# Splitting most of the weights during the first group, with GpSimd for the low parts of the first four pieces

## The reference

```python
# 1. attention with decay: batch 4, 8 heads, 768 tokens, head size 48
cur = einsum('bhd,bhe->bhde', u * kt, vt)
y[:, :, t] = einsum('bhd,bhde->bhe', rt, state + cur)
state = w * state + einsum('bhd,bhe->bhde', kt, vt)
# 2. gated layer on x: 3072 tokens x 384, hidden size 1536
x = (sigmoid(x @ w_gate) * (x @ w_val)) @ w_out
# 3. each token goes to one of 8 experts (hidden size 1024)
logits = normalised(x) @ normalised(expert_emb).T / tau
e = argmax(logits);  out = softmax(logits)[e] * (relu(x @ w1[e]) @ w2[e])
```

## Time and profile before

| what | value |
|---|---|
| median of 3 runs | 874.27 us (873.17 to 874.39) |
| the profiled execution's own time | 874.71 us |
| its span, first to last instruction | 873.0 us |
| TensorE busy (matmul) | 846.8 us, 97% of the span |
| VectorE, ScalarE, GpSimd busy | 430.7, 303.2, 426.2 us |
| 0 to 16 us | TensorE busy 11.22 of 16.00, mean clock 0.89 |
| 16 to 55.6 us | TensorE busy 32.02 of 39.60, mean clock 0.68 |
| 55.6 to 128.8 us (group 0) | TensorE busy 73.09 of 73.20, mean clock 0.96 |
| 128.8 to 196 us | TensorE busy 67.20 of 67.20, mean clock 1.00 |

### The profile page before, as it was taken

One profiled execution on the slowest core, in us unless ns is written; L12 is line 12 of the kernel. 1 busy time (PEld: TensorE's weight loads), 2 busy tenths in 40 slices (PEclk: granted clock), 3 DMA queues, 4 the chain that ended last, 5 costly groups with the idle time before them and its releaser, 6 DMA issues.

```text
span 873.0 us, 20522 instructions
## 1 busy us (share of the span) xinstructions
PE 846.8 (97%) x7508; PEld 798.4 (91%) x7509; DVE 430.7 (49%) x1051; ACT 303.2 (35%) x622; POOL 426.2 (49%) x452
## 2 busy tenths in 40 slices
PE   7799999999999999999999999998999999999995
PEld 6689999999999999999999999987899989989995
DVE  6755456456446446445545542386356266265100
ACT  1532232233233233223223223423544444454442
POOL 3656417417417417416516513245566476466544
PEclk8869999999999999999999999999999999999999
DMA  9532202302302212212212200236344344354110
GB/s 279 198 117 76 84 29 84 93 21 85 88 26 84 71 43 85 78 35 84 71 41 87 65 33 19 73 108 174 111 142 144 114 150 143 101 159 138 50 35 29
DMA packets 76021, 79.68 MB, mean 91 GB/s; under 512 B 5720, under 2 KB 73248, under 8 KB 75952
## 3 DMA queue, kind: packets, MB, share of 16 engines
q1 hardware_dynamic: 62800, 57.93, 22.0%
q10 hardware_dynamic: 9216, 9.55, 3.9%
q0 software_dynamic: 3936, 11.23, 3.4%
HBM read 67.47 MB, written 12.01 MB: 91 GB/s over the span
## 4 chain that ended last, share of the span: by engine, by line
PE 89%; DVE 5%; POOL 2%; issue 2%; DMA 1%; ACT 1%; SPq 0%; POOLq 0%; ACTq 0%; DVEq 0%
PE ps L1261 35%; PE ps L1278 17%; PE ps L1374 13%; PE ps L1359 13%; PE ps L1382 3%; PE ps L1187 2%; PE ps L1210 1%; PE ps L1194 1%; PE ps L1218 1%; PE ps L1339 1%; PE ps L1224 1%; POOL weights L626 1%; DMA staged<-in_moe_w 1%; DVE weights L1015 1%; DMA w_col<-in_w 0%
## 5 line engine op out<-in xcount | busy, mean ns | idle before, releaser
L1261 PE MATMUL ps<-x_groups,weights 128*128 128x384 f32 x1728 | 317.9, 340 | 0.0
L1261 PEld LDWEIGHTS ps<-x_groups,weights 128*128 128x128 f32 x1728 | 299.9, 189 | 1.9
L567 POOL TENSOR_TENSOR hT<-gate,hT 128x384 fp32r<-128x384 f32 x96 | 104.3, 1089 | 138.4 <-ACT hT L705 138.4
L1278 PE MATMUL ps<-weights,hT 128*128 128x392 f32 x864 | 160.6, 344 | 0.0
L1278 PEld LDWEIGHTS ps<-weights,hT 128*128 128x128 f32 x864 | 152.6, 188 | 0.4
L1374 PE MATMUL ps<-weights,hT 128*128 x672 | 124.1, 339 | 1.7 <-ACT h_f L807 1.7
L1359 PE MATMUL ps<-weights,x_groups 128*128 (+1 forms) x504 | 122.8, 397 | 1.2 <-DVEq L1020 1.0
L1027 DVE TENSOR_TENSOR gate<-ps,gate 128x384 f32<-128x384 f32 x96 | 53.6, 558 | 136.8 <-PE ps L1261 130.3
L1374 PEld LDWEIGHTS ps<-weights,hT 128*128 128x128 f32 x672 | 115.9, 188 | 1.9 <-issue 1.9
L1359 PEld LDWEIGHTS ps<-weights,x_groups 128*128 128x128 f32 x504 | 92.6, 188 | 20.4 <-issue 1.7
L1013 DVE CAST weights<-staged 128x768 fp32r<-128x768 f32 x56 | 50.3, 898 | 102.2 <-PE ps L1359 55.1
(11 more groups left out here) (181 smaller groups left out, 1001.9 us busy)
## 6 DMA issues: line engine op xcount, KB each, us to landing
staged<-in_moe_w SPq DMA_DIRECT2D x60, 384.0 KB
r_in<-routed ACTq DMA_DIRECT2D x30, 192.5 KB
rk_raw<-in_rt SPq DMA_DIRECT2D x21, 256.0 KB, 3.6
rk_raw<-in_kt SPq DMA_DIRECT2D x21, 256.0 KB, 3.9
r_in<-in_r SPq DMA_DIRECT2D x21, 192.0 KB, 2.4
k_in<-in_k SPq DMA_DIRECT2D x21, 192.0 KB, 2.5
v_in<-in_v SPq DMA_DIRECT2D x21, 192.0 KB, 2.3
first_raw<-in_moe_w_out SPq DMA_DIRECT2D x6, 384.0 KB, 14.0
```

What stands on the lines that cost most here:

```text
L567: g.tensor_tensor(hT_lo[:, f, :], gate[:, f % 2, :], hT_hi[:, f, :].bitcast(F32), ALU.subtract).then_inc(hlo_ready, 1)
L1261: ins = te.matmul(ps[:, bank[f % 2], 0:GT], wt[:, c, fs], x[:, half, c, :], start=(c == 0 and m == 0), stop=(c == KC - 1 and m == 2))
L1278: ins = te.matmul(ps[:, BX2[i], 0:XW], h[:, f, ts], wt[:, f, :], start=(f == 0 and m == 0), stop=(f == FC - 1 and m == 2))
```

## The change

1. The host passes a transposed w_out as one more input; six pieces t0 to t5 of it are loaded and TensorE reads the logit chunks from them directly. The transposes of w_out on TensorE and ScalarE's copies are gone. The o pieces are still loaded, so six more pieces of 384 KB are.
2. Before the first hidden step only g0, v0, g1 and v1 are split: high parts on ScalarE, low parts on GpSimd (early_lo): g0 after tile 0's attention, v0 after tile 1's, g1 and v1 after tile 2's.
3. The other 14 pieces are split in group 0, behind the hidden steps that HI_AT (ScalarE), LO_AT (VectorE) and LO_O_AT (GpSimd) name.
4. Rooms are reused: PIECES gives each piece a room, and SyncE waits until the piece that was in it is used up. The loads of tiles 3 to 5 stand between those of the pieces. ScalarE issues the inputs of tiles 0 to 2 (18 DMAs) ahead of all its other work.
5. The order of the start is written out anew, without FIRST; VectorE scales k of the next tile ahead of stage 2. GpSimd makes k_tok ahead of its wait for y_turned, in every tile.
6. In group 0, TensorE waits for g and v of a pair of steps at even f, for o pieces in the projection.

The orders in which pieces are loaded (with the room of each: s the staging buffers, h the room of h_f, x beside the first group's x, l in the second half of h) and split:

```diff
+    PIECES = [("g", 0, "s0"), ("v", 0, "s1"), ("t", 0, "l0"), ("t", 1, "l1"), ("t", 2, "l2"), ("t", 3, "x0"),
+              ("t", 4, "x1"), ("t", 5, "x2"), ("g", 1, "h"), ("v", 1, "l3"), ("g", 2, "l4"), ("v", 2, "l5"),
+              ("g", 3, "s0"), ("v", 3, "s1"), ("o", 0, "x0"), ("o", 1, "x1"), ("o", 2, "x2"), ("v", 4, "l3"),
+              ("g", 4, "h"), ("g", 5, "l4"), ("v", 5, "l5"), ("o", 3, "s0"), ("o", 4, "s1"), ("o", 5, "h")]
...
+    HI_SEQ = [("g", 0), ("v", 0), ("g", 1), ("v", 1), ("g", 2), ("o", 0), ("o", 1), ("v", 2), ("o", 2), ("g", 3),
+              ("v", 3), ("v", 4), ("o", 3), ("g", 4), ("o", 4), ("g", 5), ("v", 5), ("o", 5)]
+    LO_SEQ = [("g", 0), ("v", 0), ("g", 1), ("v", 1), ("g", 2), ("v", 2), ("g", 3), ("v", 3), ("v", 4), ("g", 4),
+              ("g", 5), ("v", 5)]
+    HI_AT = {1: "g2 o0", 2: "o1 v2", 3: "o2 g3", 4: "v3", 5: "v4 o3", 6: "g4 o4", 7: "g5", 8: "v5 o5"}
+    LO_AT = {1: "g2", 3: "v2", 4: "g3 v3", 5: "v4", 7: "g4 g5", 8: "v5"}
+    LO_O_AT = {2: "o0 o1", 3: "o2", 6: "o3 o4", 8: "o5"}
+    LO_POOL = LO_SEQ[:4]
...
+        def lo_count(kind, j):
+
+            if kind == "o":
+                return piece_done_o, j + 1
+            n = LO_SEQ.index((kind, j)) + 1
+            return (piece_done_first, n) if (kind, j) in LO_POOL else (piece_done, n - len(LO_POOL))
```

SyncE's queue; load_pieces waits until the piece before in the same room is used up:

```diff
+            load_pieces(PIECES[:17])
+            fetch(sp, 0, 3)
+            fetch_v(sp, 0, 3)
+            load_pieces(PIECES[17:20])
+            fetch(sp, 0, 4)
+            load_pieces(PIECES[20:21])
+            fetch_v(sp, 0, 4)
+            load_pieces(PIECES[21:23])
+            fetch(sp, 0, 5)
+            fetch_v(sp, 0, 5)
+            load_pieces(PIECES[23:])
```

GpSimd, in the loop over f behind attention(f - 1) and hidden_step(f), in hidden_step, and at the start behind each tile:

```diff
                     hidden_step(G, f)
+                    if G == 0:
+                        for kind, j in pieces_at(LO_O_AT, f):
+                            _, raw, hi, lo = piece(kind, j)
+                            pool.wait_ge(piece_hi, HI_SEQ.index((kind, j)) + 1)
+                            g.tensor_tensor(lo, raw, hi.bitcast(F32), ALU.subtract).then_inc(piece_done_o, 1)
...
+                if G == 0 and f in (6, 8, 10):
+                    pool.wait_ge(*lo_count(*{6: ("v", 4), 8: ("g", 5), 10: ("v", 5)}[f]))
...
+            def early_lo(kind, j):
+                _, raw, hi, lo = piece(kind, j)
+                pool.wait_ge(piece_hi, HI_SEQ.index((kind, j)) + 1)
+                g.tensor_tensor(lo, raw, hi.bitcast(F32), ALU.subtract).then_inc(piece_done_first, 1)
...
+                if i < 2:
+                    early_lo("gv"[i], 0)
+            early_lo("g", 1)
+            early_lo("v", 1)
```

ScalarE (make_hi waits for the piece to land and casts it; it also stands in the loop over f, by HI_AT) and, in its stage 3 of tile 3, a wait for o2, whose room the next group's x takes:

```diff
+                    if isinstance(T, int) and T == TPG:
+                        act.wait_ge(*lo_count("o", 2))
...
+            for c in range(TPG):
                 fetch(act, 0, c, waits=False)
                 fetch_v(act, 0, c, waits=False)
...
+            make_hi("g", 0)
+            make_hi("v", 0)
+            for i in range(TPG):
+                attention(0, i, i, 3, 0)
+            make_hi("g", 1)
+            make_hi("v", 1)
```

VectorE, in the loop over f behind attention(f - 1), and its start:

```diff
                         attention(*att_of(b, half, f - 1), 1 - half)
+                    if G == 0:
+                        for kind, j in pieces_at(LO_AT, f):
+                            make_lo(kind, j)
...
+            def make_lo(kind, j):
+                _, raw, hi, lo = piece(kind, j)
+                dve.wait_ge(piece_hi, HI_SEQ.index((kind, j)) + 1)
+                ve.tensor_tensor(lo, raw, hi.bitcast(F32), ALU.subtract).then_inc(piece_done, 1)
+
+            attention(0, 0, 0, 1, 0)
+            for i in range(TPG):
+                if i + 1 < TPG:
+                    scale_k(0, i + 1)
+                attention(0, i, i, 2, 0)
+                if i + 1 < TPG:
+                    scale_r(0, i + 1)
+                attention(0, i, i, 3, 0)
+                if i + 1 < TPG:
+                    attention(0, i + 1, i + 1, 1, 0)
```

TensorE, its hidden step and its start:

```diff
-                if f * P % GCOLS == 0:
-                    pe.wait_ge(piece_done, split_by(ORDER.index(("v", f * P // GCOLS))))
+                if G == 0 and f * P % GCOLS == 0:
+                    for kind in "gv":
+                        pe.wait_ge(*lo_count(kind, f * P // GCOLS))
...
+            for i in range(TPG):
+                attention(0, i, i, 1)
+                if i == 0:
                     turn_embeddings()
...
+                    pe.wait_ge(enT_ready, 1)
+                for c in range(4 * i, 4 * i + 2):
+                    logit_columns(c)
+                attention(0, i, i, 2)
+                for c in range(4 * i + 2, 4 * i + 4):
+                    logit_columns(c)
+                attention(0, i, i, 3)
+                keep_clock(BX2[1], 4)
             hidden_step(0, 0, 0, first=True)
```

More of the change, by code:

```diff
@@ L61, in fused_kernel @@
     NWO, NWG = FC // OCH, FF // GCOLS
-    PRE = NWO + 2 * NWG
     XH = 256
@@ L210, in fused_kernel @@
         enT_ready = sem("enT_ready")
-        first_in = [sem(f"first_in{n}") for n in range(NFIRST)]
+        room_arrived = {room: sem("arrived_" + room) for room in dict.fromkeys(ROOM_OF.values()) if room[0] != "s"}
         staged_in = [sem("staged_in0"), sem("staged_in1")]
@@ L349, in fetch_v @@
             if waits:
-                before = 1 if T == 2 else T
+                before = 1 if T == TPG else T
                 eng.wait_ge(y_psum, before)
@@ L455, in _, with load_pieces @@
                          u.rearrange("h d -> (h d)").partition_broadcast(P)).then_inc(small_in, 16)
[L457 to L463, removed]
+            def load_pieces(pieces):
+                for kind, j, _ in pieces:
+                    src, raw, _, _ = piece(kind, j)
+                    if tenant_before(kind, j) is not None:
+                        sp.wait_ge(*consumed(*tenant_before(kind, j)))
+                    sp.dma_start(raw, src).then_inc(landed(kind, j)[0], 16)
+            load_pieces(PIECES[:17])
[9 more added lines that the diff above has]
+            load_pieces(PIECES[23:])
+            for T in range(2 * TPG, NT):
                 fetch(sp, *divmod(T, TPB))
@@ L527, in attention @@
                 if stage == 0:
+                    start = isinstance(T, int) and T == 0
                     pool.wait_ge(*arrival(T))
-                    if not (isinstance(T, int) and T == 0):
-                        pool.wait_ge(y_turned, T)
+                    if start:
+                        pool.wait_ge(pow_ready, 1)
+                    else:
                         pool.wait_ge(scores, T)
-                    if isinstance(T, int) and T == 0:
+                    g.tensor_tensor(k_tok[:, :, 0:D], k_t[:, :, :], pow_tok[:, :, :], ALU.mult).then_inc(k_tok_ready, 1)
+                    if start:
                         pool.wait_ge(small_in, 48)
@@ L744, in split_first, with make_hi @@
                     s_.copy(hi, expert_view(0, i, chunks)).then_inc(piece_hi, 1)
-            for c in range(2):
+            def make_hi(kind, j):
+                _, raw, hi, _ = piece(kind, j)
+                piece_arrived(act, kind, j)
+                s_.copy(hi, raw).then_inc(piece_hi, 1)
+            for c in range(TPG):
                 fetch(act, 0, c, waits=False)
@@ L1227, in logit_columns @@
             def logit_columns(c):
-                pe.wait_ge(wo_copied, c + 1)
+                raw = piece("t", c // 2)[1]
+                if c % 2 == 0:
+                    piece_arrived(pe, "t", c // 2)
                 for q in range(KC):
-                    for part in HALVES:
-                        ins = te.matmul(ps[part, BX, c * E:(c + 1) * E], gate[:, c % 2, q * P:(q + 1) * P][:, part],
-                                        enT[:, q, :], start=(q == 0), stop=(q == KC - 1))
+                    for n, part in enumerate(HALVES):
+                        at = c % 2 * P + n * HP
+                        ins = te.matmul(ps[part, BX, c * E:(c + 1) * E], raw[:, q, at:at + HP], enT[:, q, :],
+                                        start=(q == 0), stop=(q == KC - 1))
                 ins.then_inc(wo_logit, 1)
```

204 lines of the change are left out of this document (89 added, 115 removed).

## The result

The changed kernel takes 876.38 us (median of 20 runs, 873.86 to 880.22) against 873.38 (870.76 to 877.85): 3.0 us slower, ratio 1.0034, 95% interval 1.0020 to 1.0049. The forecast was 873.6: the sum of −0.7 put to the profiled execution, less its 0.4 above the median then shown. The time lies in the stated range; its direction was given 0.35. The two profiled executions differ by less, 875.92 against 874.71, because each lies on the other side of its own median.

What follows compares the result with a forecast made beforehand. TensorE was taken to bound the kernel from 55.6 us on, GpSimd's weight splitting to pace the start. −13.7+5.4+4.8+2.8 = −0.7 us against 874.7 gave 874.0, less 0.4 for the median 873.6; range 866.5 to 879.

Steps and rivals of the forecast that it cites:

- The start, −13.7: Before group 0's first hidden step: that step starts at 41.9 instead of 55.63 us; bounds −15.5 and −10.
- so no other engine can take much of this away: Start, tile 1 to 2: GpSimd's multiply and wait are under 1 us shorter than VectorE's and TensorE's path to y.
- tile 1 to 2, 8.3: Start: masks and bonus sum 2.05, multiply 1.6, v0's low part 1.83, k_tok 1.7, matmuls 1.15, ending at 34.9.
- The first hidden step at the lower clock, no term: Group 0, first hidden step: expected at the lower clock as before, so no gain or cost.
- Step 4, +5.4 (2.4 to 6.4): Group 0: TensorE stalls before step 4 for v2's low part, behind stage 2 of tile 3 on VectorE; +5.4 us.
- Step 6, no term: Group 0: no TensorE stall priced before step 6; only VectorE's product of step 6 late, by 0.5 to 2.2, taken 1.2.
- Step 8, +4.8: Group 0: TensorE stalls before step 8 for g4's low part, behind stage 2 of tile 4; +4.8 us, bounds 2.4 and 5.8.
- Clock, +2.8: Group 0, behind the stalls before steps 4 and 8: each clock fall costs 0 to 2.9, taken 1.4; +2.8 us together.
- GpSimd is in time: Group 0: both stalls only 2.4 and too short for the clock; −8.9 us, 865; chance 0.12.
- Tile 2's inputs are late: Start: tile 2's inputs land after 28.6; at 3 us late +2.3, 876.6; chance 0.15.
- both stalls at their upper bounds and slow refill: Group 0, steps 4 and 8: stalls 12.2 together plus 5 for the clock; +3.5 us, 877.8; chance 0.13.
- rival 4: Start doesn't shorten because something else paces the tiles; counted only as part of "Tile 2's inputs are late", no own chance.

Runs made afterwards that it cites:

- vector_first_four: Changed kernel with VectorE instead of GpSimd making the low parts of g0, v0, g1 and v1; ratio 1.0031 to the kernel before.
- no_fill: Changed kernel without the clock-keeping matmuls at the end of each of the start's three tiles; 879.26 us, ratio 1.0050 to the kernel before.
- fill_stalls: Changed kernel plus 36 and 24 calls of the clock-keeping matmul before the waits of steps 4 and 8; ratio 1.0004 to the kernel before.
- lows_earlier: Changed kernel with VectorE's low parts of v2 behind step 2 (was 3) and g4 behind 6 (was 7); 868.38 us, ratio 0.9923 to before.
- w_out_spread: Changed kernel with GpSimd's low part of o1 moved from step 2 to 3 and o4 from 6 to 7; ratio 1.0011 to the kernel before.
- fill_short: Changed kernel plus 24 and 14 calls of the clock-keeping matmul before the waits of steps 4 and 8; ratio 0.9981 to the kernel before.
- low_after_scale: Changed kernel with GpSimd waiting for VectorE's scaling of the next tile's r before g0's and v0's low parts; ratio 1.0041 to the kernel before.
- one_low_spread_vector: Changed kernel with one VectorE low part a step, w_out's spread on GpSimd, VectorE making the first four; 864.37 us, ratio 0.9876 to before.

## Why the prediction was wrong

The sum was −0.7 us and +3.0 was measured (+2.0 in this pair of traces, at the end of the first group's hidden steps). The large terms held to 1.6 us or better; what turned the sign is a start 1.6 us later than worked out and a third stall of 1.6 that had no term, with step 4 at its upper bound (0.9), against 2.0 that the first step gave.
- *The start, −13.7.* Measured −12.1. The step "so no other engine can take much of this away" failed. I followed GpSimd; but in this trace TensorE's own queue is the chain of tiles 1 and 2. Per tile it holds 24 matmuls twice (L1313, the logit chunks, 1.4 us each) and eight filling ones (L1387, 1.7) among the others, all at the lower clock. Of the three terms of the start the one that failed is "tile 1 to 2, 8.3": VectorE's first mask operations of the two tiles begin 9.5 us apart, the tile before and the tile behind are within 0.2 of theirs. The chain has no GpSimd in it, and vector_first_four, which takes GpSimd's four pieces away, doesn't start sooner; no_fill, which takes 1.7 us out of TensorE's queue there, brings the 9.5 to 7.8, and fill_stalls, with the upper clock there, to 7.7. In the six other traces with this start GpSimd does come in ahead of tile 1, by another way than the one I priced: VectorE's scaling of r, which begins during GpSimd's low part of g0, takes 3.0 to 4.2 us, and TensorE waits 0.4 to 1.7 for it. VectorE's two rows, and the chain of waits through tile 1, of the changed kernel:

```profile
26.82 0.36 DVE L960 TENSOR_TENSOR A_room<-ps,Z 128x192 f32<-128x192 f32 x1 [1.89 <-PE ps L1273]
...
36.33 0.36 DVE L960 TENSOR_TENSOR A_room<-ps,Z 128x192 f32<-128x192 f32 x1 [2.56 <-PE ps L1273]
```

```profile
26.75 1.38 PE ps L1313 x24
...
32.66 1.71 PE ps L1387 x8
```

- *The first hidden step at the lower clock, no term.* It gave −2.0: 3.96 us from start to product instead of 5.97, since the upper clock came within 2 us of its start. I had expected it to run as before; this gain was not foreseen, and it hid about half of the 4.1 us of the other errors.
- *Step 4, +5.4 (2.4 to 6.4).* Measured 6.3. Mechanism and rows were right, the size near the upper bound: g2's low part took 1.75 us and v2's 2.18, where I had 0.95 and 1.96, and that makes the 0.9; o0's and o1's took 3.73 together, as worked out. lows_earlier shows that the place of v2's low part is the cause, w_out_spread that GpSimd's lateness is 1.7 us of it.
- *Step 6, no term.* Measured 1.6, and this is the step of the reasoning that failed outright: I put g3's and v3's low parts down as lateness of VectorE's products and overlooked that TensorE itself waits for v3's before step 6. Two in a row beside GpSimd's k_tok take 3.48 instead of 1.9. At 1.9 they would have been done at 73.6, as TensorE reached its wait (73.8), so it is the contention that made this wait cost anything.
- *Step 8, +4.8.* Measured 4.5. Right: lows_earlier, which moves g4's low part, leaves 0.5 of it.
- *Clock, +2.8.* Measured 1.3 and 1.5 as slow steps in the trace; fill_short returns 2.8. Right, and by experiment; that the size fits so well is in part luck, since the same two falls cost 4.9 in low_after_scale.
- *Other waits, none.* Some 0.4 us between steps 8 and 11, not followed up.

Together −12.1−2.0+6.3+1.6+4.5+2.8+0.4 = +1.5, the rest to 2.0 being some 0.1 us more at each stall, 0.3 between steps 5 and 7, and rounding. Each error is small beside the terms, but terms of −14 and +13 cancel, and the sign hung on them. The rival "GpSimd is in time" was wrong. "Tile 2's inputs are late" was too: by the trace VectorE scaled tile 2's k at 28.75 with no idle time before it. Of "both stalls at their upper bounds and slow refill", only the stall before step 4 came near its bound. None of the rivals had the third stall, and rival 4, "something else paces the tiles", had no price of its own; that some of their sums (876.6, 877.8) lie near 876.4 is chance, and so is that the time lies in the range.

Open: why the medians differ by 1 us more than the first groups of the two traces. The profiled executions are one each; kernels with the same start begin their first hidden step anywhere from 41.8 to 45.1, and the same two falls of the clock cost 2.8 to 4.9 us.

## What to carry to other kernels

Work that is moved into a stretch where the bounding engine is never idle costs mostly by its place, not by its amount: put it where nothing that the bounding engine waits for next stands behind another wait (here the same work in other steps was worth 10 us, and spread to one piece a step 12 to 14, a difference near the noise). When a start is priced, follow the queue of every engine, the filling instructions and the lower clock included, before naming the one that paces it. A stall of several us on TensorE is paid again in the clock behind it, and matmuls that compute nothing inside the stall give that part back. One profile is not enough to price a start: here traces of kernels with the same start differed by up to 3.3 us.

## What the runs showed of the hardware

One VectorE operation with two SBUF inputs (the scaling of tile 1's r, 0.69 us alone) took 2.1 to 4.2 us when it began during GpSimd's low part of g0, which also has two SBUF inputs; when it began during GpSimd's k_tok (vector_first_four, one_low_spread_vector) it took 1.2 and 1.5. In lows_earlier it outlasted three of them in a row; GpSimd's instructions there:

```profile
21.89 1.83 POOL L673 TENSOR_TENSOR weights<-staged,weights 128x768 fp32r<-128x768 f32 x1
23.66 1.01 POOL L580 TENSOR_TENSOR k_tok<-first_room,pow_tok 128x384 f32<-128x384 f32 x1
24.61 1.00 POOL L587 TENSOR_TENSOR bonus<-first_room 128x384 f32<-128x384 f32 x1
25.69 1.34 POOL L589 TENSOR_TENSOR bonus<-bonus,u_tok 128x384 f32<-128x384 f32 x1
```

VectorE's ran from 21.94 to 26.17 (above). It was not done when the first ended at 23.7, nor when the second and the third did. In the changed kernel the same operation was done at 24.34, after one. So the price of such contention is not one instruction of the other engine, and it is not the same from run to run. The Trainium skill, GPSIMD Engine Reference, section 1 Specifications, says that GpSimd shares its SBUF interfaces with VectorE and that VectorE instructions with two SBUF inputs contend. The runs agree on that.
